# Attention on three engines in an order written out call by call, with the sums of keys into the state taken out of the group products

## What is computed

```python
mag = np.sqrt(a_re * a_re + a_im * a_im)
scale = np.minimum(mag, 0.999) / (mag + 1e-06)
a_re_n, a_im_n = (a_re * scale, a_im * scale)
for t in range(S):
    new_re = ar * S_re - ai * S_im
    new_im = ar * S_im + ai * S_re
    S_re, S_im = (new_re + kv, new_im)          # kv = outer(k_t, v_t)
    y[:, :, t] = np.einsum('bhd,bhde->bhe', q[:, :, t], S_re)
```

## Time and profile before

| | us |
|---|---|
| median of 3 runs | 535.58 |
| lowest, highest | 534.78, 536.91 |
| profiled execution | 535.94 |
| its span | 534.0 |

### The profile page before, as it was taken

One profiled execution on the slowest core, in us unless ns is written; L12 is line 12 of the kernel. 1 busy time (PEld: TensorE's weight loads), 2 busy tenths in 40 slices (PEclk: granted clock), 3 DMA queues, 4 the chain that ended last, 5 costly groups with the idle time before them and its releaser, 6 DMA issues.

```text
span 534.0 us, 9866 instructions
## 1 busy us (share of the span) xinstructions
PE 456.1 (85%) x3712; PEld 412.5 (77%) x3712; DVE 348.6 (65%) x551; ACT 270.4 (51%) x425; POOL 43.9 (8%) x50
## 2 busy tenths in 40 slices
PE   0538887889981079999999998999999999999995
PEld 0327677689871079999999997988989999899985
DVE  2589596595317057777767776777747877487751
ACT  5997769863433056666665663333333333334312
POOL 2000000000015850000000000000021000110002
PEclk9968998999995569999999999999999999999999
DMA  8980010010002497666676664333324332230001
GB/s 315 421 328 2 3 4 1 2 4 3 2 2 89 150 329 229 191 197 189 190 218 207 201 197 117 110 99 108 90 87 144 95 118 89 80 98 1 0 1 61
DMA packets 27149, 63.75 MB, mean 119 GB/s; under 512 B 7894, under 2 KB 9430, under 8 KB 27100
## 3 DMA queue, kind: packets, MB, share of 16 engines
q1 hardware_dynamic: 25564, 58.34, 34.2%
q0 software_dynamic: 1536, 4.74, 2.3%
HBM read 58.28 MB, written 4.76 MB: 118 GB/s over the span
## 4 chain that ended last, share of the span: by engine, by line
PE 74%; DVE 6%; DMA 5%; ACT 4%; issue 4%; POOL 3%; SPq 2%; DVEq 0%; POOLq 0%; ACTq 0%
PE banks L1116 16%; PE banks L1118 16%; PE banks L1117 16%; PE banks L1126 8%; DMA vv<-v_rows 4%; PE banks L1127 4%; PE banks L978 3%; POOL rows_by_slot L391 3%; PE banks L936 2%; PE banks L966 2%; PE banks L997 2%; PE banks L969 2%; PE banks L1000 1%; PE banks L1110 1%; PE banks L1020 1%
## 5 line engine op out<-in xcount | busy, mean ns | idle before, releaser
L856 DVE TENSOR_TENSOR w_lo<-raw_early,w_hi 128x768 fp32r<-128x768 f32 x84 | 80.0, 956 | 30.5 <-ACT w_hi L552 29.5
L597 ACT ACTIVATE g_hi<-g_all 128x512 fp32r<-128x512 f32 x48 | 30.4, 632 | 118.8 <-DVE g_all L909 118.8
L552 ACT ACTIVATE w_hi<-raw_early 128x768 fp32r<-128x768 f32 x84 | 70.3, 843 | 32.2 <-PE banks L1127 32.0
L1116 PE MATMUL banks<-w_hi,g_hi 128*128 128x384 f32 x192 | 65.1, 339 | 0.5 <-DVE g_lo L911 0.5
L1118 PE MATMUL banks<-w_hi,g_lo 128*128 128x384 f32 x192 | 65.0, 339 | 0.0
L1117 PE MATMUL banks<-w_lo,g_hi 128*128 128x384 f32 x192 | 64.9, 338 | 0.0
L1126 PE MATMUL banks<-h_hi_lo,w_hi 128*128 128x448 f32 x192 | 63.9, 378 | 0.7 <-DVE h_hi_lo L872 0.7
L911 DVE TENSOR_TENSOR g_lo<-g_all,g_hi 128x512 fp32r<-128x512 f32 x48 | 33.2, 693 | 44.3 <-ACT g_hi L597 44.3
L1116 PE MATMUL banks<-ys_hi,w_hi 128*128 128x512 f32 x144 | 56.1, 390 | 1.4 <-DVE ys_lo L886 1.4
L1118 PE MATMUL banks<-ys_hi,w_lo 128*128 128x512 f32 x144 | 57.1, 397 | 0.0
L1117 PE MATMUL banks<-ys_lo,w_hi 128*128 128x512 f32 x144 | 56.8, 394 | 0.0
(11 more groups left out here) (146 smaller groups left out, 941.5 us busy)
## 6 DMA issues: line engine op xcount, KB each, us to landing
raw_early<-weights SPq DMA_DIRECT2D x84, 384.0 KB, 3.6
raw_late<-weights SPq DMA_DIRECT2D x28, 384.0 KB, 3.1
xq<-q_rows SPq DMA_DIRECT2D x3, 776.0 KB, 17.0
xq<-rows_by_slot SPq DMA_DIRECT2D x12, 194.0 KB, 4.1
kk<-k_rows SPq DMA_DIRECT2D x3, 768.0 KB, 18.1
vv<-v_rows SPq DMA_DIRECT2D x3, 768.0 KB, 19.5
aa<-a_re_rows SPq DMA_DIRECT2D x2, 768.0 KB, 11.0
th<-a_im_rows SPq DMA_DIRECT2D x2, 768.0 KB, 12.3
```

What stands on the lines that cost most here:

```text
L552: A(wh[:, slot, :], raw[slot], ACT.Copy).then_inc(w_hi, 1)
L597: A(gh[:, c % GBUF, :], gg[:, c % GBUF, :], ACT.Copy).then_inc(g_hi, 1)
L856: TT(wl[:, slot, :], raw[slot], wh[:, slot, :].bitcast(F32), ALU.subtract).then_inc(w_lo, 1)
L1116: MM(o, lhsT=whi, rhs=mhi, start=first, stop=False)
```

## The change

Both `attend` functions, ACT's loop over `step` and `LOGITS_AT` go. In their place each of the three engines has one straight list of calls for all three frames. `apply_group` is split: it keeps the products into YB, and `add_group` has the eight products into UB, so that each has a place of its own in PE's list. The instructions on PE are the same 3902 rows in another order. Waits that stood between frames (`qkv_here`, `phi_ready`, `small_dma`, `exp_ready`) move into the calls. `x_transpose(0)` waits for `phi_ready` 6, since xT shares its memory with `carry`. `k_evacuate` on ACT and `first_q_evacuate` wait for `transposed`. In the last frame `add_group` is called for groups 0 to 3 alone, as before.

```diff
@@ ACT @@
             def k_evacuate(f, g):
+                act.wait_ge(transposed, 8 * f + (g + 1))
                 act.wait_ge(scored, KT_FREE + 8 * f + (g + 1 - 2))
...
-            for step in range(8 * NF + 3):
-                f, s = step // 8, step % 8
...
+            logs(2)
+            inverses(2)
+            q_evacuate(0, 2)
+            correction(2)
+            squares(3)
+            q_evacuate(0, 3)
+            angle(2)
...
+            exps(1, 1)
+            logs(3)
+            q_evacuate(0, 6)
+            sin_cos(1, 0)
+            q_evacuate(0, 7)
+            y_evacuate(0, 1)
+            inverses(3)
...
@@ DVE @@
-            for f in range(NF - 1):
-                attend(f, f + 1)
-            attend(NF - 1, None)
+            k_evacuate(0, 2)
+            rotate(0, 3)
+            mask_scores(0, 1)
+            tangent(2)
+            rotate(0, 4)
+            clip_log(2)
+            k_evacuate(0, 3)
+            correct_log(2)
+            state(0, 0)
+            mask_scores(0, 2)
+            k_evacuate(0, 4)
+            rotate(0, 5)
+            rotate(0, 6)
+            squared_sum(3)
...
+            k_evacuate(0, 6)
+            carry_angle(1, 1)
+            mask_scores(0, 4)
+            mask_scores(0, 5)
...
+            rotate(2, 0)
+            phase(2, 1)
@@ PE @@
+            def values_here(f, g):
+                if g == 0:
+                    pe.wait_ge(qkv_here, f + 1)
+                    if f == 0:
+                        pe.wait_ge(phi_ready, 2)
...
+            def add_group(f, g):
+                values_here(f, g)
+                if g % 2 == 0:
+                    pe.wait_ge(state_out, U_FREE + 6 * f + (-1, 1, 2, 3)[g // 2])
+                for i in range(G4):
+                    h = g % 2 * G4 + i
+                    MM(UB[0:SINE, h * D:(h + 1) * D], lhsT=kt[:, g % 4, i, 0:SINE], rhs=values(f, g, i),
+                       start=True, stop=True)
+                    x = MM(UB[SINE:DP, h * D:(h + 1) * D], lhsT=kt[:, g % 4, i, SINE:DP], rhs=values(f, g, i),
+                           start=True, stop=True)
+                x.then_inc(added, 1)
...
             def x_transpose(t):
+                if t == 0:
+                    pe.wait_ge(phi_ready, 2 * NF)
...
+            transpose_group(0, 4)
+            L_sums(1, 0)
+            add_group(0, 2)
+            add_group(0, 3)
+            score_group(0, 3)
...
+            score_group(0, 5)
+            transpose_group(0, 7)
+            score_group(0, 6)
+            Th_sums(1, 1)
...
+            transpose_group(1, 7)
+            x_transpose(0)
+            apply_group(1, 5)
+            add_group(1, 7)
...
+            x_transpose(10)
+            apply_group(2, 6)
+            apply_group(2, 7)
+            tile_logits(9)
+            x_transpose(11)
+            tile_logits(10)
+            tile_logits(11)
```

More of the change, by code:

```diff
@@ L495, in _ @@
             table(LOGS)
[L496 to L505, removed]
+            square(0)
+            square(1)
+            logs(0)
+            logs(1)
+            inverses(0)
+            inverses(1)
+            correction(0)
+            correction(1)
+            angle(0)
+            angle(1)
             squares(2)
@@ L728, in shift_state @@
                    ALU.mult).then_inc(state_out, 1)
[L730 to L780, removed]
+            re_square(0)
+            abs_square(0)
+            re_square(1)
+            abs_square(1)
+            tangent(0)
+            tangent(1)
+            clip_log(0)
+            clip_log(1)
+            correct_log(0)
@@ new lines, in _ @@
+            shift_state(0, 0)
+            mask_scores(0, 6)
+            mask_scores(0, 7)
+            state(0, 3)
+            clip_log(3)
+            tangent(3)
+            correct_log(3)
+            shift_state(0, 1)
+            rotate(1, 3)
+            mask_scores(1, 0)
+            mask_scores(1, 1)
+            scale(1, 1)
+            state(1, 0)
+            rotate(1, 4)
+            mask_scores(1, 2)
+            rotate(1, 5)
+            state(1, 1)
+            carry_angle(2, 0)
@@ new lines, in _ @@
+            apply_group(1, 0)
+            apply_group(1, 1)
+            transpose_group(1, 3)
+            add_group(1, 2)
+            score_group(1, 2)
+            add_group(1, 3)
+            L_sums(2, 1)
+            apply_group(1, 2)
+            score_group(1, 3)
+            transpose_group(1, 4)
+            add_group(1, 4)
+            Th_sums(2, 0)
+            transpose_group(1, 5)
+            apply_group(1, 3)
+            add_group(1, 5)
+            score_group(1, 4)
+            score_group(1, 5)
@@ new lines, in _ @@
+            add_group(1, 6)
+            transpose_group(1, 6)
+            Th_sums(2, 1)
+            apply_group(1, 4)
+            score_group(1, 6)
+            transpose_group(1, 7)
+            x_transpose(0)
+            apply_group(1, 5)
+            add_group(1, 7)
+            transpose_group(2, 0)
+            score_group(1, 7)
+            x_transpose(1)
+            apply_group(1, 6)
+            transpose_group(2, 1)
+            tile_logits(0)
+            apply_group(1, 7)
+            x_transpose(2)
@@ new lines, in _ @@
+            score_group(2, 0)
+            add_group(2, 0)
+            add_group(2, 1)
+            transpose_group(2, 2)
+            tile_logits(1)
+            x_transpose(3)
+            tile_logits(2)
+            score_group(2, 1)
+            transpose_group(2, 3)
+            x_transpose(4)
+            apply_group(2, 0)
+            score_group(2, 2)
+            transpose_group(2, 4)
+            apply_group(2, 1)
+            add_group(2, 2)
+            x_transpose(5)
+            tile_logits(3)
@@ new lines, in _ @@
+            score_group(2, 3)
+            tile_logits(4)
+            transpose_group(2, 5)
+            score_group(2, 4)
+            apply_group(2, 2)
+            add_group(2, 3)
+            x_transpose(6)
+            apply_group(2, 3)
+            x_transpose(7)
+            tile_logits(5)
+            transpose_group(2, 6)
+            score_group(2, 5)
+            apply_group(2, 4)
+            x_transpose(8)
+            score_group(2, 6)
+            tile_logits(6)
+            transpose_group(2, 7)
@@ L1092, in _ @@
+            apply_group(2, 5)
+            x_transpose(9)
+            tile_logits(7)
+            score_group(2, 7)
+            tile_logits(8)
+            x_transpose(10)
[5 more added lines that the diff above has]
+            tile_logits(11)
             pe.wait_ge(onehot, 1)
```

239 lines of the change are left out of this document (167 added, 72 removed).

## The result

The changed kernel takes 521.76 us in the median of 4 runs (521.50 to 523.34), the kernel before 535.29 beside it (534.78 to 536.91): the ratio is 0.975, with a 95% interval of 0.973 to 0.977, so 13.5 us faster. Forecast were 523.5 us and 12.1 us. Two executions are left out of all that follows, since they were far slower than the rest: one of the kernel before (684 us) and one of the kernel before with extra transposes (1179 us).

The account below looks back on a forecast made before the run. PE's own work was taken to bound the attention once order gaps go: 41.2 + 100.1 + 5 waits (1.2, 0.5, 1.6, 0.3, 1.8) + 1.0 = 147.7 against 159.8, so about 523.5 us; range 519.0 to 531.0.

Parts of the forecast that it names:

- What bounds it: Attention from 41.2 us: PE has 100.1 us of work in 118.6 us; 18.5 us are gaps and half clock.
- The front: Last frame's front: `squared_sum(3)` and `logs(3)` move earlier, so `L_sums(2, 0)` comes near 80 us, 16 us early.
- The first gap: At `L_sums(1, 0)`, 49.3 us: PE waits 1.2 us for `correct_log(2)`, plus 0.5 us for half clock.
- The new wait: Frame 0, `score_group(0, 6)`: PE waits about 1.6 us for `mask_scores(0, 4)`, which stands behind `carry_angle(1, 1)` on DVE.
- The tail: After the last product: two copies of 0.49 us and handovers leave PE idle 1.8 us.
- The sum: End of the last logits: 146.7 us plus 1.0 for unseen waits makes 147.7, against 159.8; 12.1 us gained.
- The split: `add_group` may run while `apply_group` waits for its mask; no instructions change, any gain already counted as fewer gaps.
- A: The waits move: half the removed gaps, 6 us, come back across the engines, giving 529.5 us; chance 0.16.
- B: No change: frame 1's gaps stay behind ACT's tables and `sin_cos`, only the tail is won, 534.5 us; chance 0.05.
- C: Slower: `x_transpose(0)` waits for `phi_ready` 6, losing time if `phase(2, 1)` ends after 117.6 us; chance 0.04.
- D: Denser than the strides: PE packs as the LDWEIGHTS share says, 22 us gained in the attention, 513 us; chance 0.02.

Follow-up runs that it names:

- the run that swaps two calls: Changed kernel with `mask_scores(0, 4)` ahead of `carry_angle(1, 1)` in DVE's list: 520.89 us, ratio 0.973.
- the second experiment: Changed kernel with every `add_group` directly behind its `apply_group` again and nine DVE calls moved to avoid a circle of waits: 546.11 us, ratio 1.019.
- the run with the late front: Changed kernel with the elementwise front of the last frame put back late in ACT's, DVE's and PE's lists: 532.78 us, ratio 0.995.

## Why the prediction was right, and where its sizes were off

*What bounds it.* Right. PE's work at full clock from the start of group (0, 2) was put at 100.1 us, from strides. The windows show 101.6 us from 41 us and 0.5 us ahead of it: 102.1. The sum was 2% too short. Counted from start to start in the changed kernel's timeline, without the marked waits, transposes took 21.4 us (20.2 in the sum), scores 23.0 (22.5), products and sums into UB 35.5 (34.5), and the sums of blocks 11.3 (12.2). Such strides can hold short waits that the timeline doesn't mark, so how much of the 2.0 us is work and how much waiting stays open. The middle value for `x_transpose`, 0.43, had no second row beside 0.39; it took 0.45. That LDWEIGHTS gave 100.7 was luck: the same scaling makes 87.87 / (25.31 / 28) = 97.2 us of the changed kernel's nine stretches, in which PE was busy 101.6. And PE is full from 75 us on, as the run with extra transposes confirms.

*The front.* Right to about a microsecond: `squared_sum(3)` at 53.0 (54 forecast), `logs(3)` at 58.8 (60), `L_sums(2, 0)` at 79.8 (80), `L_sums(2, 1)` at 86.9 (88), `Th_sums(2, 1)` at 99.4 (99). But "After that PE has as much left as before, and it is PE-bound" leans on the order: in the old loop the same early front gives 5.2 us and not 12.

*The first gap.* The wait was 1.05 us, 1.2 forecast. The 0.5 us for half clock was not paid: `L_sums(1, 0)` took 1.56 us, about the 1.53 of the earlier trace rows, where it had taken 2.48 on the chain. The clock stayed at 1.00.

*The new wait.* 1.62 us for DVE's mask at 65.6 us, 1.6 forecast at 65. It was taken away by the run that swaps two calls. The 0.3 us at `L_sums(2, 0)` for `correct_log(3)` did not come: `correct_log(3)` ended at 78.43 us, 1.4 us ahead of PE.

*The tail.* Forecast 1.8 us idle. The windows show 0.27 us ahead of the last transposes and some 0.1 behind: the logits of tile 10 fill the time of the copy. That is the largest miss among the waits, 1.4 us.

*The sum.* Forecast: 41.2 + 100.1 + 5.4 + 1.0 = 147.7. Measured: 40.5 + 102.1 + 3.1 = 145.7, with 1.05 + 1.62 + 0.4 of waits. So the start 0.7 earlier, the work 2.0 more, the waits 3.3 less, the 1.0 for waits that a walk doesn't see among them. The earlier start is scatter between executions, as shown above, and owes nothing to the order. Without it the forecast of the attention was off by 1.3 us, from two misses that partly cancel: 2.0 too little work and 3.3 too much waiting. That the sum came so near is in part luck.

*The split.* The step that failed is "A gain from it isn't excluded but is already counted, as fewer gaps", read as: of no account in itself. Alone it is worth nothing in the loop (535.04, 530.0), and that half holds. But the order of the change rests on it: with the adds behind their products and nine DVE calls moved for it, the lists take 546.1 us. The forecast of the whole was not hurt, for its walk followed the split order call by call.

*The rivals.* A and B fell: no gap of over 2 us is left in frame 1. C fell: `phase(2, 1)` ends at 102.96 us, far ahead of 117.6, and `x_transpose(0)` starts at 103.76 without a wait. The margin is only 0.8 us; in both kernels with joined adds `x_transpose(0)` did wait, 1.13 us. D fell too, with 521.8 against 513. The Trainium skill (Perfetto Trace Analysis, Identifying the Most-Contended Engine) takes LDWEIGHTS' share, beside the share of peak arithmetic, as the distance to full. From 75 to 89 us PE never rests and that share is 11.52 of 14, 82%; the 18% left are no room, since 3.5 us more of work cost 3.7 us.

*What stays open.* How the 24 us of the second experiment divide between the joined adds and the nine DVE calls that moved with them; the joined adds without the moved calls would make the engines wait in a circle, and the moved calls without the joined adds weren't tried. What the early front alone is worth in the new order, with `logs(3)` behind `y_evacuate(0, 2)`. And whether moving the first logits is worth the 0.3 us that one pair of traces shows.

## What to carry to other kernels

Where an engine is full in one stretch and has gaps in another, count its whole work from dense strides and list the gaps with their releasers. Then bring the head of the longest chain across engines forward into the stretch that starves, and count the parts of such a change together: here the early front was worth 5 us in the old loop, and the fine order 8 us on top of it. Whether the two are worth more together than each alone isn't shown, since the run with the late front had a wait of its own. When you put a call back to test it, check what it now stands ahead of. Separate calls that need no wait from those that do before writing such an order, and ask with a little extra work without use whether the engine that you take for the bound really is.

## What was not expected of the hardware

The granted clock took a gap of 1.05 us at 49 us without a mark (1.00 before, in and behind it), while with the gap of 2.20 us at nearly the same place it was 0.84 in that stretch and 0.91 from 53 to 63 us. The changed kernel's gap of 1.62 us left 1.00 as well, and so did gaps of 2.08 us at 67 us (changed kernel with extra transposes) and of 2.04 us at 91 us (front late). Behind the 3.55 us of the run with the late front it was 0.50 from 78 to 80 us, the lower of its two levels. These are single executions, not a law.
